# Gate logits of an attention and mixture-of-experts kernel: three bfloat16 parts instead of fp32 products

## What is computed

```python
# 4 x 768 = 3072 tokens; heads 8 x 64 = 512 columns; 8 experts
x = attention(q, k, v)            # sinks of 4 keys, window of 128 keys
h = x @ w_in                      # 512 -> 2048
x = (h - tanh(h)) @ w_out         # 2048 -> 512; called x2 in the kernel

logits = x @ w_gate + modality_bias[modality_id]   # 512 -> 8
e_idx = argmax(logits, axis=1)
gate_w = softmax(logits)[e_idx]
for e in range(8):                # top-1 routing
    mask = e_idx == e
    h = np.maximum(x[mask] @ w1[e], 0.0)           # 512 -> 1024
    out[mask] = gate_w[mask, None] * (h @ w2[e])   # 1024 -> 512
```

## Time and profile before

| | |
|---|---|
| time, median of 3 runs | 1068.89 us (1068.62 to 1070.78) |
| span of the profiled execution, first to last instruction | 1067.3 us |
| own time of the profiled execution | not given apart; the median stands 1.6 us over its span |
| PE busy | 986.2 us, 92% of the span |
| DVE busy | 699.5 us, 66% |
| ACT busy | 612.0 us, 57% |
| POOL busy | 400.9 us, 38% |
| mean granted TensorE clock | 0.973 of 2.4 GHz |

### The profile page before, as it was taken

One profiled execution on the slowest core, in us unless ns is written; L12 is line 12 of the kernel. 1 busy time (PEld: TensorE's weight loads), 2 busy tenths in 40 slices (PEclk: granted clock), 3 DMA queues, 4 the chain that ended last, 5 costly groups with the idle time before them and its releaser, 6 DMA issues.

```text
span 1067.3 us, 24226 instructions
## 1 busy us (share of the span) xinstructions
PE 986.2 (92%) x7776; PEld 624.8 (59%) x7776; DVE 699.5 (66%) x2464; ACT 612.0 (57%) x1425; POOL 400.9 (38%) x462
## 2 busy tenths in 40 slices
PE   1668999999999999999899999999899999899996
PEld 0534555655565565556466556555487777677773
DVE  6677977668978867877876885637665334733331
ACT  2677887757766866767676776536412224522221
POOL 4788898213344412325522341011122322232322
PEclk9767999999999999999999999999999999999998
DMA  8943113311411333211231130051025111111111
GB/s 237 328 130 71 36 36 77 120 36 37 100 36 36 65 97 71 66 36 36 40 97 36 36 65 2 1 188 31 9 43 207 53 49 44 39 41 49 49 49 38
DMA packets 25165, 75.22 MB, mean 70 GB/s; under 512 B 10032, under 2 KB 10416, under 8 KB 23536
## 3 DMA queue, kind: packets, MB, share of 16 engines
q1 hardware_dynamic: 16176, 60.65, 21.1%
q0 software_dynamic: 5728, 13.43, 3.9%
q10 hardware_dynamic: 3168, 0.02, 0.2%
HBM read 60.23 MB, written 14.12 MB: 70 GB/s over the span
## 4 chain that ended last, share of the span: by engine, by line
PE 64%; DVE 19%; issue 5%; ACT 5%; DMA 3%; POOL 2%; DVEq 1%; SPq 1%; ACTq 0%; POOLq 0%
PE h_ps L750 16%; PE acc L806 15%; PE pt_ps L1846 10%; PE h_ps L1897 5%; PE acc L1897 5%; DVE qk_top L400 3%; DVE g_raw L771 2%; PE x_out L707 2%; PE pt_ps L645 2%; PE s_ps L575 2%; PE s_ps L857 2%; DVE pt_lo L632 1%; DVE g_lo L791 1%; DMA qk_raw<-in_qk 1%; DVE ew_lo L1542 1%
## 5 line engine op out<-in xcount | busy, mean ns | idle before, releaser
L806 PE MATMUL acc<-w_out_all,g_hi 128*128 128x512 f16 x768 | 228.4, 379 | 0.0
L750 PE MATMUL h_ps<-xt_hi,w_in_all 128*128 128x384 f16 x960 | 196.7, 328 | 14.7 <-DVE g_raw L771 14.6
L806 PE MATMUL acc<-w_out_all,g_lo 128*128 128x512 f16 x384 | 145.8, 380 | 4.6 <-DVE g_lo L791 2.8
L750 PEld LDWEIGHTS h_ps<-xt_hi,w_in_all 128*128 128x128 f16 x960 | 91.7, 98 | 84.2 <-DVE g_raw L771 18.9
L628 ACT ACTIVATE pt_hi<-pt_ps 128x256 f16<-128x256 f32 (+1 forms) x192 | 69.1, 360 | 114.3 <-PE pt_ps L645 113.6
L100 POOL TENSOR_TENSOR tick<-tick 1x1 f32<-1x1 f32 x83 | 16.0, 193 | 276.2 <-ACT y L1913 118.3
L806 PEld LDWEIGHTS acc<-w_out_all,g_hi 128*128 128x128 f16 x768 | 75.0, 98 | 70.2
L791 DVE SCALAR_TENSOR_TENSOR g_lo<-g_raw,batch_scale,g_hi 128x384 f16<-128x384 f32 x128 | 90.0, 703 | 34.9 <-ACT g_hi L781 33.5
L451 POOL TENSOR_TENSOR q_stack<-qk_raw,q_stack 64x768 f16<-64x768 f32 x31 | 51.1, 1650 | 164.3 <-ACT q_stack L447 164.3
L781 ACT ACTIVATE g_hi<-g_raw,batch_scale 128x384 f16<-128x384 f32 x128 | 78.1, 610 | 39.4 <-DVE g_raw L771 39.3
L608 ACT ACTIVATE normed<-probs,row_sum 128x260 f32<-128x260 f32 (+1 forms) x192 | 92.8, 484 | 12.0 <-DVE row_sum L603 11.6
(11 more groups left out here) (310 smaller groups left out, 2109.0 us busy)
## 6 DMA issues: line engine op xcount, KB each, us to landing
qk_raw<-in_qk SPq DMA_DIRECT2D x62, 454.0 KB, 6.0
raw<-in_w SPq DMA_DIRECT2D x16, 512.0 KB, 7.9
v_raw<-in_v SPq DMA_DIRECT2D x4, 1536.0 KB, 9.2
x_tokens<-x SPq DMA_DIRECT2D x24, 256.0 KB, 5.7
w_in_all<-in_w_in SPq DMA_DIRECT2D x4, 1024.0 KB, 13.0
w_out_all<-in_w_out SPq DMA_DIRECT2D x4, 1024.0 KB, 12.0
x_tokens<-g_raw SPq DMA_DIRECT2D x1, 1024.0 KB, 13.7
qk_raw<-in_qk SPq DMA_DIRECT2D x2, 262.0 KB, 4.4
```

The lines of the kernel that those rows point to most:

```text
L750: mm = eng.matmul(h_of(m, f), w16[0][:, f, x * DM + k * P:x * DM + (k + 1) * P], r[:, par, k, :], start=(i == 0), stop=(i == 3 * KD - 1))
L806: mm = eng.matmul(acc[t][:, :], l[f % 2][:, t * P:(t + 1) * P], w16[1][:, f, x * DM:(x + 1) * DM], start=(f == 0 and i == 0), stop=(f == N ...
```

## The change

For 21 of the 24 tiles (all but those of `gate_last`, which keep the fp32 products):

- **Parts of the weights.** Once, on POOL at the end of window 0, `w_gate` is cut into three bfloat16 parts whose sum is the fp32 value (four small operations, so `BIAS_STEPS` is 9 and not 5).
- **Parts of the tokens.** After ACT's copy to `x2t`, POOL makes three bfloat16 parts of it, in four operations on 128x512: a cast, a subtraction, a cast, a subtraction, each waiting for the one before. ACT's next copy waits for them (`x2t_split`).
- **Products.** PE waits for the parts and does 12 bfloat16 products where there were four fp32 ones: for each of the four blocks of 128 rows, part 0 of the tokens with 24 columns (three weight parts), part 1 with 16, part 2 with 8.
- **Sum.** DVE adds up three groups of 8 columns in a reduction of its own before it adds the bias.
- **Place.** `gate_logits` moves from slots 7, 13, 19 to 8, 14, 20, and `gate_choose` from 20 to 24 to 21 to 25.

```diff
         w_gate = sb("w_gate", [P, KD, NE], F32)
+        w_gate_rest = sb("w_gate_rest", [P, KD, NE], F32)
+        w_gate_parts = sb("w_gate_parts", [P, KD, 3, NE], BF16)
+        x2t_parts = sb("x2t_parts", [P, 3, DM], BF16)
...
+                first, second, third = (w_gate_parts[:, :, i, :] for i in range(3))
+                step(eng.tensor_copy(first, w_gate[:]))
+                step(eng.tensor_tensor(w_gate_rest[:], w_gate[:], first, ALU.subtract))
+                step(eng.tensor_copy(second, w_gate_rest[:]))
+                step(eng.tensor_tensor(third, w_gate_rest[:], second, ALU.subtract))
...
             if E == "act":
                 eng.wait_ge(q["x2t_done"], n + 1)
-                need(eng, q["logits_ps"], n)
+                need(eng, q["x2t_split"], SPLIT_STEPS * n)
                 if n == 0:
                     eng.wait_ge(q["bias_done"], BIAS_STEPS)
                 eng.activation(x2t[:], s_bank[:, :], ACT.Copy).then_inc(q["x2t_copied"], 1)
+            if E == "pool":
+                eng.wait_ge(q["x2t_copied"], n + 1)
+                need(eng, q["logits_ps"], n)
+                step = chain(eng, q["x2t_split"], SPLIT_STEPS * n)
+                step(eng.tensor_copy(x2t_parts[:, 0, :], x2t[:]))
+                step(eng.tensor_tensor(x2t[:], x2t[:], x2t_parts[:, 0, :], ALU.subtract))
+                step(eng.tensor_copy(x2t_parts[:, 1, :], x2t[:]))
+                step(eng.tensor_tensor(x2t_parts[:, 2, :], x2t[:], x2t_parts[:, 1, :], ALU.subtract))
...
-                claim_scores(eng, (q["logits"], n + 1))
-                eng.wait_ge(q["x2t_copied"], n + 1)
+                claim_scores(eng, (q["logits"], 2 * n + 1))
+                eng.wait_ge(q["x2t_split"], SPLIT_STEPS * (n + 1))
                 for k in range(KD):
-                    mm = eng.matmul(s_bank[:, 0:NE], x2t[:, k * P:(k + 1) * P], w_gate[:, k, :], start=(k == 0), stop=(k == KD - 1))
+                    for i in range(3):
+                        mm = eng.matmul(s_bank[:, 0:(3 - i) * NE], x2t_parts[:, i, k * P:(k + 1) * P],
+                                        w_gate_parts[:, k, 0:3 - i, :].rearrange("p i e -> p (i e)"),
+                                        start=(k == 0 and i == 0), stop=(k == KD - 1 and i == 2), skip_group_check=True)
...
-                eng.tensor_tensor(logit[:, t, :], s_bank[:, 0:NE], bias_of[:, n, :], ALU.add).then_inc(q["logits"], 1)
+                step = chain(eng, q["logits"], 2 * n)
+                step(eng.tensor_reduce(logit[:, t, :], s_bank[:, 0:3 * NE].rearrange("p (i e) -> p e i", i=3), AX.X, ALU.add))
+                eng.tensor_tensor(logit[:, t, :], logit[:, t, :], bias_of[:, n, :], ALU.add).then_inc(q["logits"], 1)
...
-            if k in (7, 13, 19):
-                gate_logits(E, eng, g, (k - 7) // 6)
-            if 20 <= k < 25:
-                gate_choose(E, eng, g, (k - 20,))
+            if k in (8, 14, 20):
+                gate_logits(E, eng, g, (k - 8) // 6)
+            if 21 <= k < 26:
+                gate_choose(E, eng, g, (k - 21,))
```

More of the change, by code:

```diff
@@ L192, in front @@
                  "xt_hi_done xt_lo_done h_done tanh_done g_done g_hi_done g_lo_done x2_done evac_act evac_dve x2_st "
-                 "x2t_done x2t_copied bias_done count_set logits_ps logits early_step exp_in "
+                 "x2t_done x2t_copied x2t_split bias_done count_set logits_ps logits early_step exp_in "
                  "exp_out routed ranked slotted scattered carried").split()
@@ L252, in late_constants @@
                               table_fill[:].unsqueeze(1).to_broadcast([P, NE, NT, 2])).then_inc(q["fill_st"], 16)
-        BIAS_STEPS = 5
+        BIAS_STEPS = 9
+        SPLIT_STEPS = 4
         def token_biases(E, eng):
@@ L851, in gate_logits @@
             if E == "pe":
-                if n == 0:
-                    eng.wait_ge(q["small_in"], 48)
-                claim_scores(eng, (q["logits"], n + 1))
-                eng.wait_ge(q["x2t_copied"], n + 1)
+                claim_scores(eng, (q["logits"], 2 * n + 1))
+                eng.wait_ge(q["x2t_split"], SPLIT_STEPS * (n + 1))
                 for k in range(KD):
-                    mm = eng.matmul(s_bank[:, 0:NE], x2t[:, k * P:(k + 1) * P], w_gate[:, k, :], start=(k == 0), stop=(k == KD - 1))
+                    for i in range(3):
+                        mm = eng.matmul(s_bank[:, 0:(3 - i) * NE], x2t_parts[:, i, k * P:(k + 1) * P],
+                                        w_gate_parts[:, k, 0:3 - i, :].rearrange("p i e -> p (i e)"),
+                                        start=(k == 0 and i == 0), stop=(k == KD - 1 and i == 2), skip_group_check=True)
                 mm.then_inc(q["logits_ps"], 1)
@@ L875, in gate_choose @@
                     if part == 0:
-                        eng.wait_ge(q["logits"], TPC * (g + 1))
+                        eng.wait_ge(q["logits"], logits_count(TPC * (g + 1)))
                         need(eng, q["ranked"], g)
@@ L939, in front, with logits_count @@
         CHOOSE, SLOTTED = 10, 10
+        def logits_count(tiles):
+            return 2 * min(tiles, TPC * (NC - 1)) + max(0, tiles - TPC * (NC - 1))
         def gate_slot(E, eng, g, k):
@@ L1010, in gate_last @@
                     if t == 2:
-                        eng.wait_ge(q["logits"], n + 1)
+                        eng.wait_ge(q["logits"], logits_count(n + 1))
                     for k in range(KD):
@@ L1015, in gate_last @@
                     mm.then_inc(q["logits_ps"], 1)
-                score_readers[:] = [(q["logits"], n + TPC)]
+                score_readers[:] = [(q["logits"], logits_count(n + TPC))]
                 some(48)
@@ L1043, in join @@
             if E == "pe":
-                eng.wait_ge(q["logits"], TPC * NC)
+                eng.wait_ge(q["logits"], logits_count(TPC * NC))
                 stage_e.early_iteration(E, eng, 1, 1)
```

## The result

The changed kernel takes 1098.8 us (median of 4 runs, 1096.7 to 1102.2) against 1069.4: ratio 1.0278, with a 95% interval of 1.026 to 1.0297. The forecast was 1075.9 with 1070 to 1082 as its range. The direction is right and the size is not; 23 us are to be explained.

A forecast was written before the change was run, and what follows sets the result against it. PE was taken to bound windows 1 to 6. Products -9.0, collisions +1.0, slot 8 +13.0 and clock +2.0 gave +7.0 us: span 1067.3 to 1074.3, time 1075.9 with the median 1.6 over the span; range 1070 to 1082.

The forecast's parts named there:

- Products, -9.0: Windows 1 to 7: twelve bfloat16 products take 0.40 us a tile, not 0.855 us for fp32; 9.0 us saved in all.
- a microsecond of PE work taken out of these windows is a microsecond of time: Windows 1 to 6: PE, busy 495.9 of 508.0 us, sets the time, but for what waits for `g_raw` eat.
- I cost this at nothing net: DVE's extra reduction per tile, 172 ns, costs nothing net: DVE is 77% busy and the logits leave the odd slot.
- Contention with `g_lo`, +1.0: DVE's `g_lo` slowed beside POOL's new operations, 1.53 us against a mean of 0.70: 1.0 us over 21 tiles.
- The stall, +13.0: Window 7, tile 0: POOL's parts queue behind the gathers, PE waits at the logits, slot 8 starts 13.0 us later.
- the clock, +2.0: Behind window 7's wait PE runs at half speed at first, one or two stretches: 2.0 us.
- The clock in windows 1 to 6: PE's clock was read as full, 2.4 GHz, in windows 1 to 6; no cost was put on it there.
- the collisions bite: Rival: products at 56 ns and `g_lo` late at a tight place in most windows, 1080 to 1086 us; chance 0.13.

The follow-up runs named there:

- experiment 7: Kernel before with 12 bfloat16 products and DVE's reduction in the old slots, ACT writing the only token part, none on POOL: 1063.6 us against 1068.5, ratio 0.996.
- experiment 15: Changed kernel with POOL's gathers behind window 7's first parts and the choice's multiplication by -8 folded into the addition of `iota_e`: 1073.5 us, ratio 1.0051.
- experiment 1: Changed kernel with POOL's wait for the x2 stores and its three gathers moved behind the parts of window 7's first tile: 1084.1 us, ratio 1.0151.
- experiment 4: Kernel before, fp32 products kept, with only the slots changed: logits in 8, 14, 20 and choice in 21 to 25: 1081.4 us, ratio 1.012.
- 11: Kernel before with logits in 8, 14, 20, choice from 21, and the multiplication by -8 folded into the `iota_e` addition: 1069.3 us against 1068.2, ratio 1.0011.
- experiment 2: Changed kernel with the logits in slots 9, 15 and 20 and the choice as changed: 1085.0 us, ratio 1.0161.
- experiment 8: Kernel before plus POOL's four operations per tile into unread buffers, gathers behind window 7's first parts: 1071.8 us against 1068.5, ratio 1.0037.

## Why the prediction was wrong

- **Products, -9.0.** The cost of twelve products was right and better than taken (0.32 us, not 0.40). The step "a microsecond of PE work taken out of these windows is a microsecond of time" failed where PE then had to wait for DVE: experiment 7 measured 4.9 us. In its profile the slots with the products gain 9.9 us, 2.7 go in waits right behind them, and 3.7 in one meeting with `kl_stack` and one half-speed stretch.
- **DVE's part, "I cost this at nothing net".** This is the step that made the forecast wrong. I took DVE's price as instructions times duration from idle rows (172 ns), and its 77% as slack. What the choice costs depends on what POOL does at that moment. In the changed kernel the multiplication and its neighbour met `kl_stack` in windows 1 to 5. Taking that one operation out gave 10.7 us by the times (15 against 1) and 12.8 of the 15.7 us in the profiles, half as waits and half as the clock. In experiment 4 the same move alone cost 13 us, and 11 took 12 of them away.
- **Even slots.** Also under "nothing net": I had looked at who leaves the odd slot and not at whose bank the logits need at the start of the even one. PE's waits ahead of the logits, 3.9 us, and of the scores for the longer `logit`, 2.9 us, are new. In experiment 15, where little else is left, they and 2.1 us more for `g_raw` make PE idle 8.4 us longer than before, against 5.5 us less busy: the +2.9 us that stay in windows 1 to 6. The share of the bank alone was not measured apart: experiment 2 gave 6.0 us back outside slots 23 to 25, and the meeting of the bias addition is in them.
- **Contention with `g_lo`, +1.0.** Right as far as it went: the profile of experiment 8 has 1.2 us for it, in windows 2 and 4. The rest of what the parts cost there (3.2 us by the times, 6.4 in the profile) is no `g_lo`, but a small step of the choice that met `kl_stack`, and the clock. I had asked for contention at `g_lo` alone.
- **The stall, +13.0, and the clock, +2.0.** Right: experiment 1 took 13.6 us away, and 14.1 us lie in window 7. PE stood 11.6 us and not 13.3: the stores landed 18.0 us behind the window's start (717.89 to 735.92) where it was 19.1 before, and gathers and parts took 0.65 us less.
- **The clock in windows 1 to 6.** I read "full" there and left it so. In the changed kernel it fell five times, for some 8 us of slower products. No term of the sum had a clock price for windows 1 to 6. I couldn't have read it from the waits of before: 0.8 and 1.8 us within 4 us of each other had left the clock full.
- The rival nearest to the outcome was *the collisions bite*, but it had them on `g_lo`, and its 1080 to 1086 fell short.

The Trainium skill, "SBUF — State Buffer", section "SBUF: two separate sides", states the rule that decides here: DVE and GpSimd share a pair of ports. A DVE instruction in a mode that uses both ports, or one with two SBUF inputs against a GpSimd instruction that reads SBUF, and the GpSimd instruction each take it for their whole length, and the other waits. I had weighed it and applied it to `g_lo` only, the large operation. This case's rows agree with it down to 24 elements: a small DVE operation of this kind beside POOL takes as long as POOL's still has to run (2.08 us at 244.98, to 247.06, for a POOL operation that ends at 247.03). Weighed as a price for each small SBUF step of the choice, it would have shown the slot as a risk of 2 us and not of 0.18.

What stays open: how much the bank claim at even slots costs by itself, and what decides whether the clock falls behind a pair of waits. In experiment 8 windows 2 and 4 have the same two waits, and it fell in window 2 alone.

## What to carry to other kernels

The price of a small DVE operation on SBUF is not its duration but what is left of the POOL operation beside it; so before such a step is moved, or a POOL operation is added, look in the timeline at what POOL runs in the new place, and who waits behind DVE. Look at the margin too: before, one such step started 0.06 us ahead of POOL's, and experiment 8, which shifted it by 0.07 us against POOL's, lost 2 us of DVE's time there. If PE then stands twice within a few microseconds, the clock can add 1.3 to 1.7 us. And where moving only exchanges one meeting for another, as the three starts of the choice did here, take an operation out: one 24-element step was worth 11 to 12 us in the changed placement (2.6 in the old one), more than the new products gave (4.9).

## What I had not expected of the hardware

- A 24-element `TENSOR_SCALAR` or `TENSOR_TENSOR` with all operands in SBUF takes 0.18 us alone and up to 2.20 us beside a POOL operation of 2.17 us. The same holds for the `COPY` of 128x72 (0.21 us alone, 1.17 beside POOL).
- Not every DVE operation is held. Beside the same POOL operations, reductions kept their time (128x24 in 0.18 us with POOL running for 2.0 us more; 128x1048 in 1.24), and so did operations on 128x1 (0.15 us) and those that read a PSUM bank (0.43 us for the scores).
- Products at half speed can follow waits this short: two of 1.5 us with 1.3 us of products between them, or 0.7 and 2.0 us. In the changed kernel they did in all of windows 1 to 5, in experiment 4, with nearly the same waits, only in window 5, and before, with 0.8 and 1.8 us, not at all.
- Twelve bfloat16 products of 24, 16 and 8 columns, each with a weight load of its own, run at 27 ns each.
